# Experts' second product in a fused attention and expert kernel: w2 as the stationary operand, sums turned back into rows

## What is computed

```python
# x: 1152 x 512; w1: 8 x 512 x 1024; w2: 8 x 1024 x 512; capacity 288
# disp[e] holds the rows of x whose best expert is e, in order of arrival
h = np.maximum(np.einsum('ecd,edf->ecf', disp, w1), 0.0)
y = np.einsum('ecf,efd->ecd', h, w2)
out[i] = gate_w[i] * y[expert_idx[i], pos[i]]     # for the tokens kept
```

## Time and profile before

| | us |
|---|---|
| runs (3) | median 696.5, 695.64 to 697.08 |
| the profiled execution | 699.6 |
| its span, first to last instruction | 697.9 |
| TensorE busy in the span | 631.7 |
| VectorE busy | 551.5 |
| ScalarE busy | 387.5 |
| GpSimd busy | 379.5 |

### The profile page before, as it was taken

The page is one execution under the profiler, slowest core; times in us unless marked ns, Lnnn a source line. Parts: engine busy times, 40 slices in busy tenths (PEclk is TensorE's granted clock), DMA queues, the critical chain, the costliest instruction groups (busy, mean ns, idle before and its releaser), DMA issues.

```text
span 697.9 us, 12783 instructions
## 1 busy us (share of the span) xinstructions
PE 631.7 (91%) x4180; PEld 544.3 (78%) x4180; DVE 551.5 (79%) x1009; ACT 387.5 (56%) x603; POOL 379.5 (54%) x278
## 2 busy tenths in 40 slices
PE   4678989999999999999999999989629999999996
PEld 2566977987987887888988979879528888888884
DVE  5999998989899799898899899315526667776673
ACT  2454675485585575675673863734406545556450
POOL 0779896589588688598696795940430111001111
PEclk9955797999999999999999999999859999999999
DMA  8697000000000000000000000050269455676510
GB/s 320 269 364 267 4 9 5 20 5 8 20 8 5 21 8 5 24 5 18 8 4 23 0 0 17 1 193 34 91 215 357 176 185 218 263 282 239 187 36 14
DMA packets 17789, 68.58 MB, mean 98 GB/s; under 512 B 1998, under 2 KB 6606, under 8 KB 15056
## 3 DMA queue, kind: packets, MB, share of 16 engines
q1 hardware_dynamic: 16000, 63.27, 24.0%
q0 software_dynamic: 1744, 4.73, 2.0%
HBM read 54.33 MB, written 14.45 MB: 99 GB/s over the span
## 4 chain that ended last, share of the span: by engine, by line
PE 54%; DVE 15%; issue 11%; POOL 10%; DMA 5%; ACT 4%; DVEq 0%; POOLq 0%; SPq 0%; ACTq 0%
PE p_o L1068 6%; DVE top L360 6%; PE p_a L1105 5%; DVE arena L363 5%; PE p_b L1105 4%; PE p_b L1133 4%; PE p_s L1034 4%; PE p_t L1050 3%; PE p_b L1134 3%; PE p_b L1135 3%; POOL mask L618 3%; POOL arena L622 2%; PE p_o L1288 2%; PE p_o L1290 2%; PE p_o L1289 2%
## 5 line engine op out<-in xcount | busy, mean ns | idle before, releaser
L360 DVE MAX8 top<-arena 128x8 f32<-128x576 f32 x288 | 203.8, 745 | 18.5 <-ACT arena L756 18.3
L363 DVE MATCH_REPLACE8 arena<-top,arena 128x576 f32<-128x576 f32 x216 | 158.5, 740 | 0.0
L618 POOL TENSOR_SCALAR mask<-arena,top 128x576 f32<-128x576 f32 x72 | 129.4, 1797 | 26.4 <-DVE top L360 19.0
L622 POOL TENSOR_TENSOR arena<-arena,mask 128x576 f32<-128x576 f32 x72 | 103.4, 1436 | 26.6 <-ACT arena L770 17.0
L1068 PEld LDWEIGHTS p_o<-arena,probsT 128*128 128x128 f32 x640 | 88.7, 213 | 15.0 <-ACT probsT L777 11.9
L1068 PE MATMUL p_o<-arena,probsT 128*128 128x65 f32 x640 | 90.7, 295 | 8.2 <-ACT probsT L777 8.2
L777 ACT COPY probsT<-p_t 128x640 f32<-128x640 f32 x72 | 50.4, 700 | 64.1 <-PE p_t L1050 63.9
L1050 PE MATMUL p_t<-ident,arena 128*128 128x128 f32 x360 | 59.2, 300 | 18.1 <-POOL arena L622 18.0
L1050 PEld LDWEIGHTS p_t<-ident,arena 128*128 128x128 f32 x360 | 44.8, 155 | 38.5 <-POOL arena L622 27.8
L756 ACT COPY arena<-p_s 128x576 f32<-128x576 f32 x72 | 44.2, 643 | 49.4 <-PE p_s L1034 49.4
L1034 PE MATMUL p_s<-arena,q_sb 64*128 64x224 f32 (+5 forms) x320 | 62.1, 495 | 7.2 <-DMA arena<-in_kt 4.5
(11 more groups left out here) (162 smaller groups left out, 1274.1 us busy)
## 6 DMA issues: line engine op xcount, KB each, us to landing
arena<-in_w SPq DMA_DIRECT2D x8, 2048.0 KB, 8.8
wff<-in_w SPq DMA_DIRECT2D x8, 2048.0 KB, 9.1
slot_rows<-y_now SPq DMA_DIRECT2D x1, 4626.0 KB, 27.0
wff<-in_w_out SPq DMA_DIRECT2D x1, 4096.0 KB, 20.0
wff<-in_w_in SPq DMA_DIRECT2D x1, 4096.0 KB, 15.1
wff<-slot_rows SPq DMA_DIRECT2D x8, 385.5 KB, 4.0
arena<-in_vones SPq DMA_DIRECT2D x2, 1300.0 KB, 9.5
q_sb<-in_q SPq DMA_DIRECT2D x36, 64.0 KB, 1.9
```

The lines of the kernel that those rows point to most:

```text
L360: nc.vector.max(best, src).then_inc(top_step, 1)
L363: nc.vector.match_replace(work[:, a, :], best, src, LOWEST).then_inc(top_step, 1)
L618: nc.gpsimd.tensor_scalar(mask[:], s_sb[:, t, :], top[:, t, TOP_K - 1:TOP_K], None, ALU.is_ge).then_inc(mask_made, 1)
L622: nc.gpsimd.tensor_tensor(probs[:, t % 2, :], probs[:, t % 2, :], mask[:], ALU.mult).then_inc(probs_ready, 1)
```

## The change

The down product takes w2 as the stationary operand and the hidden activations as the moving one, in the same form as the up product: two more units, 4 and 5, each of two 128-column chunks d of the model dimension, accumulated over the eight chunks f. `he_hi` and `he_lo` become one tensor `he_parts` in which high and low part of a chunk lie side by side. Units 4 and 5 write `p_pair[0]` and `p_pair[1]`, and their results are completed by `copy_cross` on ScalarE and `sum_unit` on VectorE, into `y_sum`. These have the model dimension on partitions; `turn_back` transposes them into rows in `p_oe`, four transposes after each unit. `UNITS` is 6 units per expert, and `unit_ready` and `sum_made` take the place of `he_ready` and `he_sum_made`. The completion of unit 5, the second turning back and the scaling of expert E-1 stand inside the work of expert E on each engine. On VectorE the scaling stands behind `low_he` 0.

```diff
+        y_sum = [odd_whole[:, 0:2 * SLOTS], mask[:, 0:2 * SLOTS]]
@@ def _(sp):
-                wait(sp, he_ready, 4 * E - 4)
+                wait(sp, unit_ready, UNITS * E - 2 * UNITS + UP_UNITS)
                 sp.dma_start(w1_raw[j], w1_d[e]).then_inc(w1_in[j], 16)
 
                 wait(sp, out_sent[j], 16 * NSB * turn)
                 expert_rows(e, j, r)
 
-                wait(sp, oe_ready, NSB * E - NSB)
+                wait(sp, unit_ready, UNITS * E - UNITS)
                 sp.dma_start(w2_raw[j], w2_d[e]).then_inc(w2_in[j], 16)
@@ def _(dve):
-            def sum_he(E, c, n):
+            def sum_unit(E, u, n):
 
                 m = NSB * n
...
+                wait(dve, cross_made, UNITS * E + u + 1)
+                if u < UP_UNITS:
+                    wait(dve, he_lo_made, 4 * E + u - 1)
+                    total = he_sum[u % 2]
+                else:
+                    wait(dve, oe_ready, NSB * E)
+                    total = y_sum[u % 2]
...
+            def scale_rows(E, j, turn, n):
+                wait(dve, out_sent[j], 16 * NSB * turn)
+                for s in range(NSB):
+                    wait(dve, oe_ready, NSB * E + s + 1)
+                    nc.vector.tensor_scalar(oe[j][0:n, s, :], p_oe[s][0:n, :], rows[j][0:n, s, DM:DM + 1],
+                                            None, ALU.mult).then_inc(oe_copied, 1)
+
             def expert(E, j, turn, n, more=True):
+                begin = isinstance(E, int) and E % NE == 0
+                if not begin:
+                    sum_unit(E - 1, 5, n)
                 low_w2(E, j, 0)
                 low_w2(E, j, 1)
-                sum_he(E, 0, n)
-                for c in range(1, 4):
-                    sum_he(E, c, n)
+                sum_unit(E, 0, n)
+                sum_unit(E, 1, n)
+                low_he(E, 0, n)
+                if not begin:
+                    scale_rows(E - 1, 1 - j, turn - 1 + j, n)
+                for c in range(2, 4):
+                    sum_unit(E, c, n)
                     low_he(E, c - 1, n)
                 low_w2(E, j, 2)
                 low_he(E, 3, n)
...
                 if more:
                     low_x(E + 1, n)
                     low_w1(E + 1, 1 - j)
-
-                wait(dve, out_sent[j], 16 * NSB * turn)
-                for s in range(NSB):
...
+                sum_unit(E, 4, n)
+                if not more:
+                    sum_unit(E, 5, n)
+                    scale_rows(E, j, turn, n)
@@ def _(act):
             def expert(E, j, turn, n, more=True):
+                if not (isinstance(E, int) and E % NE == 0):
+                    copy_cross(E - 1, 5, n)
                 high_w2(E, j, turn, 0)
                 high_w2(E, j, turn, 1)
                 copy_cross(E, 0, n)
...
+                copy_cross(E, 4, n)
+                if not more:
+                    copy_cross(E, 5, n)
@@ def _(pe):
+            def turn_back(E, h, n):
+                m = NSB * n
+                wait(pe, sum_made, UNITS * E + UP_UNITS + h + 1)
+                if h == 0:
+                    wait(pe, oe_copied, NSB * E)
+                pe.sem_inc(tensor_waits, 1)
+                for s in range(NSB):
+                    for d in range(2):
+                        at = P * (2 * h + d)
+                        last = nc.tensor.transpose(p_oe[s][0:n, at:at + P],
+                                                   y_sum[h][:, m * d + n * s:m * d + n * s + n], ident[:])
+                    if h == 1:
+                        last.then_inc(oe_ready, 1)
...
-                    last.then_inc(he_ready, 1)
+                    last.then_inc(unit_ready, 1)
+                    if c == 0 and not (isinstance(E, int) and E % NE == 0):
+                        turn_back(E - 1, 1, n)
                 if more:
                     turn_rows(E + 1, 1 - j, turn + j, n)
 
-                wait(pe, oe_copied, NSB * E)
-                for c in range(4):
...
+                for h in range(2):
+                    wait(pe, sum_made, UNITS * E + UP_UNITS + h - 1)
+                    for d in (2 * h, 2 * h + 1):
+                        cols = slice(P * d, P * d + P)
+                        bank_d = p_pair[h][:, d % 2, :]
+                        for f in range(FC2):
+                            if d == 0 and f % 2 == 0:
+                                wait(pe, he_lo_made, 4 * E + f // 2 + 1)
+                                wait(pe, w2_lo_made, 4 * E + f // 2 + 1)
+                            both_he = he_parts[:, 2 * m * f:2 * m * f + 2 * m]
+                            high_he = he_parts[:, 2 * m * f:2 * m * f + m]
+                            if f < FC2 - 1:
+                                mm(bank_d[:, 0:2 * m], w2_hi[:, f, cols], both_he, start=(f == 0), stop=False)
+                                mm(bank_d[:, 0:m], w2_lo[j][:, f, cols], high_he, start=False, stop=False)
...
+                    last.then_inc(unit_ready, 1)
+                turn_back(E, 0, n)
+                if not more:
+                    turn_back(E, 1, n)
```

More of the change, by code:

```diff
@@ L46 @@
 LAG = 4
+UP_UNITS, UNITS = 4, 6
 def build(nc, q_in_d, kt_in, v_in, w_in_d, w_out_d, wg_d, w1_d, w2_d, out):
@@ L103, in build @@
         he_at = x_at + 2 * KC * SLOTS
-        he_hi = over("he_hi", wff, he_at, [FC2 * SLOTS])
-        he_lo = over("he_lo", wff, he_at + FC2 * SLOTS, [FC2 * SLOTS])
+        he_parts = over("he_parts", wff, he_at, [FC2 * 2 * SLOTS])
         q_sb = sb("q_sb", [P, H // 2, P])
@@ L201, in build @@
         xe_ready, x_hi_made, x_lo_made = sem("xe_ready"), sem("x_hi_made"), sem("x_lo_made")
-        he_ready, he_hi_made, he_lo_made = sem("he_ready"), sem("he_hi_made"), sem("he_lo_made")
-        cross_made, he_sum_made = sem("cross_made"), sem("he_sum_made")
+        unit_ready, he_hi_made, he_lo_made = sem("unit_ready"), sem("he_hi_made"), sem("he_lo_made")
+        cross_made, sum_made = sem("cross_made"), sem("sum_made")
         oe_ready, oe_copied = sem("oe_ready"), sem("oe_copied")
@@ L552, in low_w2 @@
                                         w2_hi[:, part, :].bitcast(F32), ALU.subtract).then_inc(w2_lo_made, 1)
-            def sum_he(E, c, n):
+            def sum_unit(E, u, n):
                 m = NSB * n
[L557 to L563, removed]
+                wait(dve, cross_made, UNITS * E + u + 1)
[5 more added lines that the diff above has]
+                    total = y_sum[u % 2]
+                nc.vector.tensor_tensor(total[:, 0:2 * m].rearrange("p (b s) -> p b s", b=2),
+                                        p_pair[u % 2][:, :, 0:m],
+                                        cross[u % 2][:, 0:2 * m].rearrange("p (b s) -> p b s", b=2),
+                                        ALU.add).then_inc(sum_made, 1)
@@ L565, in low_he @@
             def low_he(E, c, n):
+                m = NSB * n
                 wait(dve, he_hi_made, 4 * E + c + 1)
-                part = slice(4 * n * c, 4 * n * c + 4 * n)
-                nc.vector.scalar_tensor_tensor(he_lo[:, part], he_sum[c % 2][:, 0:4 * n], 0.0,
-                                               he_hi[:, part].bitcast(F32), ALU.max,
+                part = he_parts[:, 4 * m * c:4 * m * c + 4 * m].rearrange("p (f v s) -> p f v s", f=2, v=2)
+                nc.vector.scalar_tensor_tensor(part[:, :, 1, :],
+                                               he_sum[c % 2][:, 0:2 * m].rearrange("p (f s) -> p f s", f=2), 0.0,
+                                               part[:, :, 0, :].bitcast(F32), ALU.max,
@@ L584, in expert @@
                     low_w1(E + 1, 1 - j)
-                wait(dve, out_sent[j], 16 * NSB * turn)
-                for s in range(NSB):
-                    wait(dve, oe_ready, NSB * E + s + 1)
-                    nc.vector.tensor_scalar(oe[j][0:n, s, :], p_oe[s][0:n, :], rows[j][0:n, s, DM:DM + 1],
-                                            None, ALU.mult).then_inc(oe_copied, 1)
+                sum_unit(E, 4, n)
+                if not more:
+                    sum_unit(E, 5, n)
+                    scale_rows(E, j, turn, n)
             low_x(0, ROUNDS[0][1])
@@ L948, in high_w1 @@
                 wait(act, w1_in[j], 16 * (turn + 1))
-                wait(act, he_ready, 4 * E)
+                wait(act, unit_ready, UNITS * E - UNITS + UP_UNITS)
                 for c in range(4):
@@ L975, in high_w2, with copy_cross @@
                         act.wait_ge(second_round_known, 1)
-                    wait(act, oe_ready, NSB * E)
+                    wait(act, unit_ready, UNITS * E)
                 nc.scalar.copy(w2_hi[:, 2 * c:2 * c + 2, :], w2_raw[j][:, 2 * c:2 * c + 2, :]).then_inc(w2_hi_made, 1)
-            def copy_cross(E, c, n):
+            def copy_cross(E, u, n):
                 m = NSB * n
[L982 to L986, removed]
+                wait(act, unit_ready, UNITS * E + u + 1)
+                wait(act, sum_made, UNITS * E + u - 1)
+                nc.scalar.copy(cross[u % 2][:, 0:2 * m].rearrange("p (b s) -> p b s", b=2),
```

(17 more changed lines are left out.)

1 line of the change is left out of this document (added).

## The result

The changed kernel takes 751.3 us (median of 6 runs, 749.7 to 757.2) against 696.2 us of the kernel before (6 runs): a ratio of 1.080, 95% interval 1.077 to 1.083, that is 55 us more. The profiled execution took 756.6 us with a span of 754.8 us, 56.9 us more than the span of before. It is one of the two long ones of the six (spans 754.8 and 755.5 us, the other four 747.9 to 750.1), so the trace shown here is some 5 us above the median.

The account below looks back on a forecast made before the run. TensorE was taken to bound the experts' stage, with a scaling-scatter-reload cycle without slack. 696.5 + 63.4 us (six pauses 49, clock 15.6, splits and bare end about 7, shorter work -7, small ones) gave 760 us, range 742 to 770.

Parts of the forecast that it names:

- rival 1: TensorE's clock does not fall in the pauses, or comes back at once; pauses stay: 744 us, chance 0.12.
- The order of the waits: Between experts: late scaling, scatter, row load, then TensorE's transposes; TensorE waits 8.1 us for rows, six times.
- T to the scaling: From T, the end of a previous expert's unit 5, to VectorE's scaling behind `low_he` 0: 7.2 us.
- Scaling to transposes: From VectorE's scaling through scatter and row load to TensorE's transposes: unchanged 11.0 us, 0.3 shorter or 1 longer.
- The two loads of weights behind the rows: On SyncE's queue, w2's and next w1's loads follow the rows; w2 covered, 8.8 us against more than 12.
- The clock: TensorE's clock halves after each pause for rows, costing 2.6 us each, 15.6 us for six.
- The cycle: Period of an expert between scalings, pause and clock loss included: 30.9 us where it was 21.1.
- The last expert: Expert 7: down product catches VectorE's splits, ends at T+22.3; bare completion follows, scaling at T+24.35, 754.6 us.
- T+14.8: Start point in the sum for expert 7's product end; VectorE's last low part of w2 was put at T+14.6.
- The start and the end: Expert 0's unit 5 ends at 545.1 us, before 544.9; the 6.7 us after the last scaling stay.
- Rival 2: VectorE's splits, not the rows, pace each expert at 22.3 us: median 708.6 us, chance 0.04.
- Rival 3: TensorE's down-product saving, 0.9 us per expert, decides and the kernel is faster: 691 us, chance 0.03.

Follow-up runs that it names:

- b_late_scale: Kernel before with its old down product, only VectorE's scaling of the previous expert moved behind `low_he` 0: 753.3 us, 1.079 to the kernel before.
- b_late_tail: Kernel before with the late scaling, plus a small buffer for gate weight and token number, so row loads skip the scatter wait: 696.8 us, 0.999.
- the filled run: Changed kernel with 28 useless identity matmuls before TensorE's wait for the rows of experts 2 to 7: 736.9 us, 1.058 to the kernel before.
- a_tail: Changed kernel with gate weight and token number copied to a small buffer, so row loads no longer wait for the scatter: 720.9 us, 1.031.
- a_tail_inter_split: Changed kernel with the small buffer, the two chunks d taken in turn per f, and `low_w2` 2 ahead of unit 3's sum: 692.7 us, 0.995.
- a_tail_inter: Changed kernel with the small buffer and the two chunks d of a down unit taken in turn for each f: 699.9 us, 1.005.
- a_early_scale: Changed kernel with VectorE's scaling moved two instructions earlier, right behind the sum of unit 0: 738.0 us, 1.057 to the kernel before.

## Why the prediction was right

It said 760 us, 742 to 770, slower with 0.96; measured were 751.3, 55 us over before where the sum had 63.4. The number by itself would not tell the forecast from rival 1: 751.3 is 8.6 us from 760 and 7.3 from 744, and the period of 29.3 us lies between the 31 and the 28 that were to tell them apart. That the mechanism was right rests on the rows and the runs. Step by step against the profiled execution, which has 56.9 us more than the earlier trace rows:

- **The order of the waits** held at every link: scaling behind `low_he` 0, scatter, rows, transposes, six times. b_late_scale and b_late_tail show this by experiment, from both sides.
- **T to the scaling**: 7.2 us foreseen; 7.2 in the chain, in which the turning back begins at 543.73, and 7.3 by the timeline, in which it begins at 543.57.
- **Scaling to transposes**: I took the 11.0 of the earlier trace rows and had it 0.3 shorter at most, for the reason that the same instructions run. It measured 10.1 in the first turn and 9.6 on the mean of six (9.3 to 10.1). This is the term that was mis-sized: 1.4 us in each turn, 8 us in all, and by as much the pauses were 6.7 us and not 8.1. In the first turn the last scatter lands in 2.7 us where it took 3.4, and over six turns the load of the rows takes 3.5 to 4.2 us where it took 4.3. The landing is counted from the start of GpSimd's instruction, which itself is shorter, 0.93 us for 1.58, as told above. The instructions are the same, but not what runs beside them. The 11.0 was also the first of the turns of before, and two later ones in its chain have 10.7.
- **The two loads of weights behind the rows** did not make the rows' load longer. That they share the DMA engines shows in w1's load, the last of the three: 12.2 us at the median to land where it took 9.1, and TensorE waits for none of them.
- **The clock**: 2.6 us foreseen for each pause, 2.4 by the medians of the filled run, 2.5 by the two traces. The mechanism was right and rival 1 was not.
- **The cycle** therefore was 29.3 us, not 30.9 (7.2 and 9.6 and 12.5, the last with the clock in it), six times: 9.2 us of the sum too much, nearly all of it from the chain of 11.0.
- **The last expert**: from the scaling of expert 6 to that of 7 I had 17.1 us, and it took 19.7. The waits for the splits are there, 1.7 and 0.7 us, but the sum did not price the clock behind them; its T+14.8 should also have been the T+14.6 worked out just before, which is small beside this (busy time by stretch, columns as above):

```profile
726.88:733.00 6.12, 4.40 (x31) 4.20 (x30) 4.83 (x9) 2.72 (x6) 1.84 (x2) 1.00 0.17 50
733.40:740.10 6.70, 6.03 (x23) 5.70 (x23) 0.92 (x1) 0.00 (x0) 0.00 (x0) 0.50 0.00 0
```

- **The start and the end** take up the rest: the first scaling came 1.4 us sooner than worked out, the end after the last scaling lasted 8.2 us where I kept the 6.7 of before. I have no explanation for this last 1.5 us; in the other runs of the changed kernel it is 6.2 to 8.3 us. So part of the closeness is luck: the errors were -1.4, -9.2, +2.6 and +1.5 us, and they cancel in part.
- **Rival 2**, splits as the pace, was put at 708.6 us. The run that makes it the case, a_tail, has 720.9. The step that failed there is the same as in the last expert: waits of 1 to 2 us were priced as themselves, without the clock.
- **Rival 3**, the product's own saving, is real: a_tail_inter_split has it. It needed the rows freed of the scatter and two changes of order, and its price, 691, is near the 692.7 measured.

The estimate of 8.5 us for a product, which took the time of a weight load from the Trainium skill (TensorE: Matmul & The Clock Gate, section LDWEIGHTS), is a little too low here: the product has 9.2 us at full clock, what the up product's rows gave.

## What to carry to other kernels

Before work is moved later in a queue, follow what its completion releases, through the scatter and into the next load of the same buffer: a step that no engine waits for can be the one that a buffer waits for. Where a small part of a buffer keeps the whole alive, copy the small part out. A saving on the busiest engine shows only once every cycle that runs through another engine is shorter than the engine's own, so compare the cycles, not the busy times. And take the length of a cycle from all its turns: here the first was the longest one in the chain, before and after.

## What was not expected of the hardware

The granted clock of TensorE fell after much less than a pause. With waits of 1.3 and 0.8 us in a stretch that was otherwise dense, busy 2.7 of 4.5 us, it was 0.50 in the 3.3 us behind, and it fell so in every expert of a_tail. With waits of 0.6 us at most, in a_tail_inter, it was 1.00 from 530 to 690 us. In between it goes either way. Expert 0 has waits of 1.0 and 0.8 us both in the changed kernel and in the run with 28 filling matmuls, and only in the second did the clock fall behind them (busy time by stretch, columns as above, the changed kernel first):

```profile
538.00:541.40 3.40, 3.40 (x25) 3.40 (x25) 3.40 (x4) 0.48 (x1) 0.00 (x0) 1.00 0.11 43
```

```profile
538.00:541.40 3.40, 3.40 (x16) 3.40 (x14) 3.40 (x4) 0.94 (x1) 0.00 (x0) 0.50 0.44 188
```

And a pause of 4.3 us cost as much half clock, 5.0 us, as one of 7.2 us, 5.1 us (the first turns of a_early_scale and of the changed kernel).
